# Layer-1 operations at new places in VectorE's and ScalarE's order, and other places for the second layer's weight blocks and three preparations

## The chip, the cores and the metric

One core of one Trainium2 chip. The number is device time in microseconds (us) for one execution; the profile divides that execution into engines: TensorE (PE, with PEld for its weight loads), VectorE (DVE), ScalarE (ACT), GpSimd (POOL) and SyncE (SP, which here only issues DMAs).

## The reference

Attention with a top-32 mask for 4 batches of 8 heads, 576 tokens, 64 numbers a head; then two feed-forward layers of 512 -> 2048 -> 512 over all 2304 tokens, with different activations:

```python
scores = scale * np.matmul(q, k.transpose(0, 1, 3, 2))
kth = np.partition(scores, -32, axis=-1)[..., -32:-31]
scores = np.where(scores >= kth, scores, -1e9)      # then softmax, then times v
# layer 1:  h = x @ w_in;  g = h if h >= 1, 0 if h <= -1, else (h + 1)**2 / 4;  x = g @ w_out
# layer 2:  h = np.maximum(x @ w_in, 0);  out = (h * h) @ w_out
```

## The kernel before

**Slots.** The attention runs in 72 slots, one for each pair of score tiles (128 queries by 576 keys). In slot n VectorE finds the 32nd largest score of each row of both tiles (`rank`): seven operations on each tile, alternately the eight largest (`max`, L920) and their replacement (`match_replace`, L922). `both(op)` issues the pair of one operation, so a slot of VectorE is `both(0)` to `both(6)`. GpSimd masks the tiles of slot n-1 in slot n (`mask`: compare with the threshold, L1083, then multiply, L1088, for each tile). PE computes the scores of slot n+1, turns the masked tiles of slot n-1 (L545) and multiplies them by v; ScalarE copies and exponentiates. VectorE also divides the product with v of slot n-2 by its row sums (`add_to_total` L928, `invert_total` L938, `scale_pv` L948).

**Steps.** The feed-forward work is cut into 18 jobs (a layer and a chunk of 256 tokens) of 16 steps (128 of the 2048 hidden numbers). Steps stand at positions q, three to a slot: q = 3n, 3n+1, 3n+2. Step k at q is `up` (12 matmuls, L613), then a chain: ScalarE's `curve` (L805 to L816), VectorE's `activate` (L977; layer 1 only), ScalarE's `split_g` (L823, L826), called by `hi_at`, GpSimd's `lo_at` (L1101); then PE's `down` at q+2 (L628, L634). The first job starts at q = 31 (slot 10) with two steps a slot; from slot 18 there are three. Jobs of layer 1 hold q 31 to 70, 103 to 168 and 233 to 280; the others are of layer 2. No step stands at q 151 and 152. Slots end with slot 73; from then on the steps run alone.

**Order of work.** Each engine runs a fixed order written out in its `slot(n)`; nothing is reordered at run time. In VectorE's slot `at(3n)` (the job's `split_x`, then `activate`) stands ahead of `both(2)`, `at(3n+1)` ahead of `both(4)`, `at(3n+2)` behind `both(6)`, and behind that VectorE's share of the weight blocks. In ScalarE's slot `hi_at(3n-1)` stands ahead of `curve_at(3n)`. In GpSimd's slot: `mask(n-1, 0)`, `lo_at(3n-1)`, `mask(n-1, 1)`, `lo_at(3n)`, `lo_at(3n+1)`, the preparation of the slot, the slot's weight blocks.

**Weights.** Numbers are held as a high and a low part. A layer has 16 blocks of 128 x 1024. A block lands in a staging buffer by DMA (SP, `stage_block`), ScalarE rounds it to the high part (L694), and GpSimd (L1074) or, for odd blocks of the second layer (`by_vector`), VectorE (L1002) subtracts for the low part. The second layer's blocks are 16 to 31; their slots are given by `W2_PER_SLOT` from slot 19 on. They land in two buffers.

**Preparations.** For each of 16 head pairs, k and q land in `kq_lo` (L324), ScalarE rounds them into `kq_hi` (L686), GpSimd subtracts (L1066), SP stores both (`restack`) and loads them again in another order. `PREP_SLOT` gives the slots. Between slots 17 and 28 `kq_lo` and `kq_hi` hold nothing that is needed, once stored.

Of the kernel before, what the change touches and what calls it, by code (L numbers as in the profile page):

```python
# [33 lines left out]
PREP_ORDER = (2, 3, 0, 1, 4, 5, 6, 7, 8, 9, 10, 11, 12, 13, 14, 15)  # L34
PREP_SLOT = (-1, 1, 3, 5, 7, 10, 12, 15, 17, 28, 30, 32, 38, 41, 44, 47)
WBLOCKS = 16
W_ORDER = [("in", 0)] + [x for j in range(7) for x in (("in", j + 1), ("out", j))] + [("out", 7)]
W1_SLOT = [-1, 0, 0, 1, 2, 2, 3, 4, 4, 5, 6, 6, 7, 8, 8, 9]
W2_PER_SLOT = (1, 2, 2, 1, 2, 2, 1, 2, 2, 1)
W_SLOT = W1_SLOT + \  # L40
# [91 lines left out]
def stage_at(i):  # L132

    return i % 4 if i < WBLOCKS else i % 2


def staged_count(i):

    return i // 4 + 1 if i < WBLOCKS else WBLOCKS // 4 + (i - WBLOCKS) // 2 + 1

# [29 lines left out]
def build(nc, kq, kq0, vv, w_raw, out):  # L170
# [8 lines left out]
    with ctx:  # L179
# [115 lines left out]
        def stage_of(i):  # L295

            return (stage[0], stage[1], xr, ys)[stage_at(i)]

# [12 lines left out]
        def _(sp):  # L311
# [8 lines left out]
            def load_kq(at):  # L320
                g = PREP_ORDER[at]
                if at:
                    sp.wait_ge(restacked, 16 * 3 * at)
                sp.dma_start(kq_lo[:, :].bitcast(F32), kq[g // PAIRS, g % PAIRS]).then_inc(kq_loaded, 16)  # L324

# [54 lines left out]
            def stage_block(i):  # L380
                if i >= WBLOCKS:
                    sp.wait_ge(w_lo_done[i % 2], i // 2)
                elif i >= 4:
                    sp.wait_ge(w_lo_done[i % 2], i // 2 - 1)
                sp.dma_start(stage_of(i)[:, :], w_raw[i]).then_inc(w_staged[stage_at(i)], 16)

# [294 lines left out]
        def _(act):  # L681
# [6 lines left out]
            def split_w(i):  # L688
                s, b = i // WBLOCKS, i % WBLOCKS
                act.wait_ge(w_staged[stage_at(i)], 16 * staged_count(i))  # L690
                if s:
                    wait_block_free(act, s, b)
                    act.wait_ge(w_moved[b], 16)
                act.activation(w_block(b)[:, 0, :], stage_of(i)[:, :], ACT.Copy).then_inc(w_hi_done, 1)  # L694

# [102 lines left out]
            def curve(k):  # L798
# [61 lines left out]
            def slot(n):  # L860
                here, nxt, before = n < SLOTS, n + 1 < SLOTS, 0 <= n - 1 < SLOTS
                q = 3 * n
                if 0 < n <= SIGNED:
                    for t in range(2):
                        keep_by_sign(n - 1, t)
                x_at(n)
                hi_at(q - 1)
                curve_at(q)
                if here:
# [40 lines left out]
        def _(dve):  # L910
# [68 lines left out]

            def at(q):  # L980
                if q in READ_AT:
                    split_x(READ_AT[q])
                if q in UP_AT:
                    activate(UP_AT[q])
# [11 lines left out]
            def split_w(i):  # L996
                if not by_vector(i):
                    return
                dve.wait_ge(w_hi_done, i + 1)
                dve.wait_ge(w_lo_done[i % 2], i // 2)  # L1000
                b = w_block(i % WBLOCKS)
                dve.tensor_tensor(b[:, 1, :], stage_of(i)[:, :], b[:, 0, :].bitcast(F32),  # L1002
                                  ALU.subtract).then_inc(w_lo_done[i % 2], 1)
# [12 lines left out]
            def slot(n):  # L1016
# [6 lines left out]

                both(0)
                if n in (NORMAL, NORMAL + 1):
                    clear_corners(n)
                both(1)
                for c in range(DIRECT):
                    if n == x_slot(c) + 1:
                        split_handed(c)  # L1030
                at(3 * n)
                behind = 1 if n < UP_POS[0] // 3 else 0
                for op in (2, 3, 4):
                    if past and op == 2 + behind:
                        add_to_total(n - 2)
                    if past and op == 3 + behind:
                        invert_total(n - 2)
                    if op == 4:
                        if past and not behind:
                            scale_pv(n - 2)  # L1040
                        at(3 * n + 1)
                    both(op)
                if past and behind:
                    scale_pv(n - 2)
                both(5)
                both(6)
                at(3 * n + 2)
                for i in range(2 * WBLOCKS):
                    if W_SLOT[i] == n:
                        split_w(i)  # L1050
                if n - 1 in SOON:
# [4 lines left out]
            for n in range(SLOTS + 2):  # L1056
                slot(n)
            for q in range(ALONE, END):
                at(q)


        @block.gpsimd
        def _(pool):
# [5 lines left out]
            def split_w(i):  # L1069
                pool.wait_ge(w_hi_done, i + 1)  # L1070
                if i >= 2:
                    pool.wait_ge(w_lo_done[i % 2], i // 2)
                b = w_block(i % WBLOCKS)
                pool.tensor_tensor(b[:, 1, :], stage_of(i)[:, :], b[:, 0, :].bitcast(F32),  # L1074
                                   ALU.subtract).then_inc(w_lo_done[i % 2], 1)
# [126 lines left out]
```

## Time and profile before

Three runs took 1258.48, 1258.61 and 1259.35 us; the median is 1258.61 us.

| | us |
|---|---|
| profiled execution, its own time | 1258.23 |
| its span, first to last instruction | 1256.4 |
| PE busy | 1193.2 (95%) |
| PEld busy | 1128.0 (90%) |
| DVE busy | 851.6 (68%) |
| ACT busy | 799.7 (64%) |
| POOL busy | 749.2 (60%) |

Busy time is the time in which at least one instruction of the engine runs; what an engine waits for inside a slot is read from its instructions in order of time. The granted clock is a share of full speed: 1.00 is 2.4 GHz and 0.50 is 1.2 GHz.

### The profile page before, as it was taken

Reading aid. Unit: us, or ns where it says so; the run is one execution under the profiler, and the core shown is the slowest. Engines: PE = TensorE matmul, PEld = TensorE weight load, DVE = VectorE, ACT = ScalarE, POOL = GpSimd, SP = SyncE. Lnnn points to the kernel's source line nnn. Section 1 sums busy time; section 2 is a strip of 40 time slices with the busy share of each in tenths; the row PEclk is TensorE's granted clock in tenths of the full one; section 3 lists DMA queues with packets and bytes.
Section 4 is the critical chain, followed back from the end, with each engine's and each line's share of the span. In section 5 each row is a group of like instructions: output and inputs, shape, how many; then the busy total and the mean of one; then the engine's idle time right before and its main releaser. Section 6 shows DMA issues by size and latency. Waiting matters only on the chain.

```text
span 1256.4 us, 24445 instructions
## 1 busy us (share of the span) xinstructions
PE 1193.2 (95%) x8760; PEld 1128.0 (90%) x8760; DVE 851.6 (68%) x1884; ACT 799.7 (64%) x1788; POOL 749.2 (60%) x620
## 2 busy tenths in 40 slices
PE   6878889999989999999999999999999999999998
PEld 3667889998889999999999999999999999999997
DVE  7999999999877799999999987868730111110000
ACT  7887666776756666767766665666554665554443
POOL 6767787878767767767666766656652222222222
PEclk9767999999989999999999999999999999999999
DMA  6766978568879932334458831456349300870000
GB/s 250 282 252 223 337 278 301 198 233 301 288 265 367 383 128 97 126 109 142 135 174 299 291 120 39 150 176 208 101 148 369 145 35 4 314 287 18 18 17 17
DMA packets 94920, 239.53 MB, mean 191 GB/s; under 512 B 7760, under 2 KB 46672, under 8 KB 82512
## 3 DMA queue, kind: packets, MB, share of 16 engines
q1 hardware_dynamic: 94800, 237.98, 53.1%
q8 instruction: 70, 1.15, 0.4%
q14 instruction: 50, 0.41, 0.1%
HBM read 166.12 MB, written 71.83 MB: 189 GB/s over the span
## 4 chain that ended last, share of the span: by engine, by line
PE 68%; POOL 12%; DVE 6%; ACT 6%; issue 5%; DMA 1%; SPq 1%; ACTq 0%; POOLq 0%
PE h_ps L613 20%; PE y_ps L634 14%; PE y_ps L628 12%; PE score_ps L613 6%; PE pv_ps L572 5%; POOL s_sb L1083 4%; PE tr_ps L545 4%; POOL prob L1088 4%; DVE top L920 3%; PE score_ps L510 3%; DVE rest L922 2%; POOL w_out L1074 1%; POOL kq_lo L1066 1%; POOL g_lo L1101 1%; PE pv_ps L584 1%
## 5 line engine op out<-in xcount | busy, mean ns | idle before, releaser
L1101 POOL TENSOR_TENSOR g_lo<-rg,g_hi 128x256 fp32r<-128x256 f32 x288 | 215.5, 748 | 407.4 <-ACT g_hi L823 227.9
L613 PE MATMUL h_ps<-xt_hi,w_in 128*128 128x256 f32 x1880 | 390.6, 291 | 2.0 <-DVE xt_lo L968 1.7
L613 PEld LDWEIGHTS h_ps<-xt_hi,w_in 128*128 128x128 f32 x1880 | 309.3, 191 | 4.3 <-issue 2.1
L920 DVE MAX8 top<-rest 128x8 f32<-128x576 f32 x432 | 304.5, 745 | 0.4
L613 PE MATMUL h_ps<-xt_lo,w_in 128*128 128x256 f32 x940 | 266.0, 283 | 0.0
L1083 POOL TENSOR_SCALAR s_sb<-s_sb,top 128x576 f32<-128x576 f32 x126 | 228.2, 1811 | 43.5 <-DVE top L920 43.5
L628 PE MATMUL y_ps<-g_hi,w_out 128*128 128x256 f32 x1152 | 231.8, 284 | 0.7 <-ACT ys L789 0.4
L922 DVE MATCH_REPLACE8 rest<-top,rest 128x576 f32<-128x576 f32 x288 | 211.5, 741 | 0.0
L634 PE MATMUL y_ps<-w_out,g_hi 128*128 128x512 f32 x576 | 203.8, 395 | 3.8 <-DVE w_out L1002 3.1
L1088 POOL TENSOR_TENSOR prob<-s_sb,prob 128x576 f32<-128x576 f32 x128 | 182.7, 1430 | 15.4 <-ACT s_sb L749 4.4
L628 PEld LDWEIGHTS y_ps<-g_hi,w_out 128*128 128x128 f32 x1152 | 189.6, 192 | 2.1 <-issue 0.6
L613 PEld LDWEIGHTS h_ps<-xt_lo,w_in 128*128 128x128 f32 x940 | 180.3, 192 | 1.5
L977 DVE SCALAR_TENSOR_TENSOR rg<-rg 128x256 f32<-128x256 f32 x144 | 83.6, 581 | 134.7 <-ACT rg L816 133.8
L628 PE MATMUL y_ps<-g_lo,w_out 128*128 128x256 f32 x576 | 162.9, 283 | 0.0
L572 PE MATMUL pv_ps<-v_sb,pt 128*128 128x65 f32 x1024 | 132.5, 287 | 0.0
L634 PEld LDWEIGHTS y_ps<-w_out,g_hi 128*128 128x128 f32 x576 | 109.3, 190 | 24.4 <-issue 4.4
L572 PEld LDWEIGHTS pv_ps<-v_sb,pt 128*128 128x128 f32 x1024 | 130.6, 207 | 0.0
L968 DVE TENSOR_TENSOR xt_lo<-xr,xt_hi 128x512 fp32r<-128x512 f32 x32 | 25.1, 826 | 151.2 <-ACT xt_hi L795 151.2
L707 ACT ACTIVATE s_sb<-score_ps 128x576 f32<-128x576 f32 x143 | 92.2, 645 | 55.5 <-PE score_ps L510 28.6
L545 PE MATMUL tr_ps<-ident,prob 128*128 128x128 f32 x576 | 96.2, 293 | 29.0 <-POOL prob L1088 26.9
L805 ACT ACTIVATE rg<-h_ps 128x256 f32<-128x256 f32 x115 | 44.2, 385 | 110.5 <-PE h_ps L613 110.2
L634 PE MATMUL y_ps<-w_out,g_lo 128*128 128x512 f32 x288 | 114.2, 396 | 0.0
(90 smaller groups left out, 2076.1 us busy)
## 6 DMA issues: line engine op xcount, KB each, us to landing
w_in<-w_scratch SPq DMA_DIRECT2D x32, 1024.0 KB, 6.5
w_out<-w_scratch SPq DMA_DIRECT2D x32, 1024.0 KB, 7.9
ks<-kq_scratch SPq DMA_DIRECT2D x46, 576.0 KB, 6.0
qs<-kq_scratch SPq DMA_DIRECT2D x152, 128.0 KB, 4.2
w_scratch<-w_in SPq DMA_DIRECT2D x16, 1024.0 KB, 8.2
w_scratch<-w_out SPq DMA_DIRECT2D x16, 1024.0 KB, 8.1
v_sb<-in_vv_dram SPq DMA_DIRECT2D x48, 325.0 KB, 5.9
stage<-in_w_dram SPq DMA_DIRECT2D x24, 512.0 KB, 4.6
```

The lines of the kernel that those rows point to most:

```text
L545: last = pe.transpose(tr_ps[t][:, P * j:P * (j + 1)], prob[n % 2][:, base + P * j:base + P * (j + 1)], ident[:, :])
L572: last = pe.matmul(pv_ps[:, V1 * t:V1 * (t + 1)], pt[:, base + P * j:base + P * (j + 1)], vb[:, V1 * (2 * j + t):V1 * (2 * j + t + 1)], st ...
L613: last = pe.matmul(h_bank(k), wi[:, f // 2, w, m, cols], x[:, m, :], start=(m == 0 and n == 0), stop=(m == KT - 1 and n == 2))
L628: last = pe.matmul(y_ps[i][:, CHUNK * (m % 2):CHUNK * (m % 2 + 1)], wo[:, f // 2, w, f % 2, P * m:P * (m + 1)], g[f % 2][:, :], start=(f = ...
L634: last = pe.matmul(y_ps[i][:, :], g[f % 2][:, P * i:P * (i + 1)], wo[:, f // 2, w, f % 2, :], start=(f == 0 and n == 0), stop=(f == FT - 1 ...
L707: act.activation(s_sb[u % 4][:, :].rearrange("p (h k) -> p h k", h=2), score_ps[:, :].rearrange("p (h k) -> p h k", h=2)[:, :, 0:HALF], AC ...
L920: dve.max(best, src[:, :]).then_inc(rank_step, 1)
L922: dve.match_replace(rest[t][:, :], best, src[:, :], LOWEST).then_inc(rank_step, 1)
L977: dve.scalar_tensor_tensor(u[:, :], r[:, :], -1.0, u[:, :], ALU.add, ALU.max).then_inc(g_done, 1)
L1083: pool.tensor_scalar(s[:, :], s[:, :], top[n % 2][:, t, TOPK - 1:TOPK], None, ALU.is_ge).then_inc(keep_done, 1)
L1088: pool.tensor_tensor(pr[:, cols], s[:, :], pr[:, cols], ALU.mult).then_inc(masked, 1)
L1101: pool.tensor_tensor(g_lo[k % 2][:, :], g_sb[k % 2][:, :], g_hi[k % 2][:, :].bitcast(F32), ALU.subtract).then_inc(g_lo_done, 1)
```

## The change

- The third step's `activate` (3n+2) moves from the end of VectorE's slot n to behind `both(0)` of slot n+1; the first from ahead of `both(2)` to behind it; the second from ahead of `both(4)` to behind it. `split_x` stays where it was.
- VectorE's low parts of weight blocks move from the end of slot n to behind `both(2)` and `activate(3n)` of slot n+1.
- In slots 2 and 3 the three operations on the product with v stand one pair of `rank` later.
- ScalarE's slot has `curve_at(3n)` ahead of `hi_at(3n-1)`, and `curve` gets a wait on ScalarE's own `split_g` two steps back in layer 2.
- The second layer's 16 blocks take nine slots (19 to 27) where they took ten (19 to 28), and land in four buffers: the two of before, `kq_lo` and `kq_hi`. The preparations of slots 28, 30 and 32 move to 29, 31 and 33. SP waits for the stored pair before it lands a block there, and for all low parts before it loads the next pair.

```diff
-PREP_SLOT = (-1, 1, 3, 5, 7, 10, 12, 15, 17, 28, 30, 32, 38, 41, 44, 47)
+PREP_SLOT = (-1, 1, 3, 5, 7, 10, 12, 15, 17, 29, 31, 33, 38, 41, 44, 47)
+IDLE_KQ = sum(s < 18 for s in PREP_SLOT)
-W2_PER_SLOT = (1, 2, 2, 1, 2, 2, 1, 2, 2, 1)
+W2_PER_SLOT = (1, 2, 2, 2, 2, 2, 2, 2, 1)
 def stage_at(i):
-    return i % 4 if i < WBLOCKS else i % 2
+    return i % 4
 def stage_of(i):
-            return (stage[0], stage[1], xr, ys)[stage_at(i)]
+            if i < WBLOCKS or stage_at(i) < 2:
+                return (stage[0], stage[1], xr, ys)[stage_at(i)][:, :]
+            return (kq_lo, kq_hi)[stage_at(i) - 2][:, 0:2 * MODEL].bitcast(F32)
 def load_kq(at):                      # SP
+                if at == IDLE_KQ:
+                    for i in range(2):
+                        sp.wait_ge(w_lo_done[i], WBLOCKS)
 def stage_block(i):                   # SP
-                if i >= WBLOCKS:
-                    sp.wait_ge(w_lo_done[i % 2], i // 2)
-                elif i >= 4:
+                if i >= 4:
                     sp.wait_ge(w_lo_done[i % 2], i // 2 - 1)
+                if i >= WBLOCKS and stage_at(i) >= 2:
+                    sp.wait_ge(restacked, 16 * 3 * IDLE_KQ)
 def curve(k):                         # ScalarE
                 if k >= 2 and JOBS[(k - 2) // FT][0] == 1:
                     act.wait_ge(g_done, CURVED[k - 2] + 1)
+                elif k >= 2:
+                    act.wait_ge(g_hi_done, k - 1)
 def slot(n):                          # ScalarE
                 x_at(n)
+                curve_at(q)
                 hi_at(q - 1)
-                curve_at(q)
 def slot(n):                          # VectorE
                 both(0)
+                activate_at(3 * n - 1)
                 both(1)
...
-                at(3 * n)
-                behind = 1 if n < UP_POS[0] // 3 else 0
-                for op in (2, 3, 4):
+                read_at(3 * n)
+                behind = 2 if n < RAW_SLOTS else 1 if n < UP_POS[0] // 3 else 0
+                for op in (2, 3, 4, 5, 6):
                     if past and op == 2 + behind:
                         add_to_total(n - 2)
                     if past and op == 3 + behind:
                         invert_total(n - 2)
+                    if past and op == 4 + behind:
+                        scale_pv(n - 2)
                     if op == 4:
-                        if past and not behind:
-                            scale_pv(n - 2)
-                        at(3 * n + 1)
+                        read_at(3 * n + 1)
                     both(op)
-                if past and behind:
-                    scale_pv(n - 2)
-                both(5)
-                both(6)
-                at(3 * n + 2)
-                for i in range(2 * WBLOCKS):
-                    if W_SLOT[i] == n:
-                        split_w(i)
+                    if op == 2:
+                        activate_at(3 * n)
+                        for i in range(2 * WBLOCKS):
+                            if W_SLOT[i] == n - 1:
+                                split_w(i)
+                    if op == 4:
+                        activate_at(3 * n + 1)
+                read_at(3 * n + 2)
```

## Rows read from the trace of the kernel before

**Rows 1.** Busy time by stage: stretch and its length, PE, PEld, DVE, ACT, POOL, PEclk, DMA
```profile
0.00:110.00 110.00, 83.53 (x335) 68.17 (x336) 100.68 (x226) 88.18 (x140) 78.55 (x46) 0.77 0.72 262
110.00:203.10 93.10, 79.42 (x641) 75.17 (x641) 91.00 (x201) 58.46 (x128) 70.97 (x51) 1.00 0.78 295
203.10:371.70 168.60, 157.55 (x1195) 149.72 (x1194) 152.06 (x319) 116.70 (x253) 133.47 (x96) 0.98 0.70 251
371.70:1256.40 884.70, 872.67 (x6595) 834.92 (x6593) 507.89 (x1143) 536.33 (x1268) 466.17 (x430) 1.00 0.45 159
```
**Rows 2.** Waits of the whole span: total us, times, longest
```profile
PE y_ps L634 <- DVE w_out L1002: 3.1, 1, 3.1
PE h_ps L613 <- DVE xt_lo L968: 1.7, 1, 1.7
```
**Rows 3.** Waits of VectorE from 26 to 60 us
```profile
DVE total L928 <- PE pv_ps L572: 1.9, 2, 1.4
```
**Rows 4.** VectorE in order of time, slots 15 to 17: start, duration, [idle before]
```profile
168.11 1.40 DVE L920 MAX8 top<-s_sb 128x8 f32<-128x576 f32 x2
...
174.59 0.76 DVE L977 SCALAR_TENSOR_TENSOR rg<-rg 128x256 f32<-128x256 f32 x1 [0.20 <-ACT rg L816]
...
179.38 1.40 DVE L920 MAX8 top<-s_sb 128x8 f32<-128x576 f32 x2
...
182.15 1.57 DVE L977 SCALAR_TENSOR_TENSOR rg<-rg 128x256 f32<-128x256 f32 x1
...
191.82 0.74 DVE L920 MAX8 top<-s_sb 128x8 f32<-128x576 f32 x1
```
**Rows 5.** GpSimd in order of time, around the start of slot 16
```profile
177.45 2.80 POOL L1066 TENSOR_TENSOR kq_lo<-kq_lo,kq_hi 128x1216 fp32r<-128x1216 f32 x1 [0.36 <-ACT kq_hi L686]
...
182.04 1.40 POOL L1088 TENSOR_TENSOR prob<-s_sb,prob 128x576 f32<-128x576 f32 x1
```
**Rows 6.** ScalarE's first operation of step 3n: slots 21, 22, 27, 28, 30
```profile
243.21 0.39 ACT L810 ACTIVATE rg<-h_ps 128x256 f32<-128x256 f32 x1 [0.21 <-PE h_ps L613]
...
257.95 0.39 ACT L810 ACTIVATE rg<-h_ps 128x256 f32<-128x256 f32 x1 [0.22 <-PE h_ps L613]
...
326.17 0.38 ACT L805 ACTIVATE rg<-h_ps 128x256 f32<-128x256 f32 x1 [2.15 <-PE h_ps L613]
...
339.78 0.38 ACT L805 ACTIVATE rg<-h_ps 128x256 f32<-128x256 f32 x1 [2.28 <-PE h_ps L613]
...
371.67 0.39 ACT L805 ACTIVATE rg<-h_ps 128x256 f32<-128x256 f32 x1 [3.02 <-PE h_ps L613]
```
**Rows 7.** GpSimd in order of time, end of slot 21
```profile
254.58 2.37 POOL L1074 TENSOR_TENSOR w_out<-stage,w_out 128x1024 fp32r<-128x1024 f32 x1 [1.16 <-ACT w_out L694]
256.92 2.95 POOL L1083 TENSOR_SCALAR s_sb<-s_sb,top 128x576 f32<-128x576 f32 x1
```
**Rows 8.** VectorE in order of time, end of slot 21
```profile
257.15 1.21 DVE L1002 TENSOR_TENSOR w_in<-stage,w_in 128x1024 fp32r<-128x1024 f32 x1
```
**Rows 9.** ScalarE's first operation of step 3n in slots 54 and 55
```profile
682.02 0.38 ACT L810 ACTIVATE rg<-h_ps 128x256 f32<-128x256 f32 x1 [1.59 <-PE h_ps L613]
...
694.70 0.39 ACT L810 ACTIVATE rg<-h_ps 128x256 f32<-128x256 f32 x1 [1.59 <-PE h_ps L613]
```
**Rows 10.** VectorE in order of time, slot 54
```profile
683.40 0.43 DVE L977 SCALAR_TENSOR_TENSOR rg<-rg 128x256 f32<-128x256 f32 x1 [0.70 <-ACT rg L816]
```
**Rows 11.** GpSimd in order of time, slot 54
```profile
682.10 0.74 POOL L1101 TENSOR_TENSOR g_lo<-rg,g_hi 128x256 fp32r<-128x256 f32 x1
682.82 1.73 POOL L1083 TENSOR_SCALAR s_sb<-s_sb,top 128x576 f32<-128x576 f32 x1
684.63 1.44 POOL L1088 TENSOR_TENSOR prob<-s_sb,prob 128x576 f32<-128x576 f32 x1
```
**Rows 12.** PE in order of time, slot 54
```profile
687.64 0.60 PE L545 MATMUL tr_ps<-ident,prob 128*128 128x128 f32 x4
```
**Rows 13.** The page's group of the layer-1 high part
```profile
L826 ACT ACTIVATE g_hi<-rg 128x256 fp32r<-128x256 f32 x144 | 60.3, 419 | 64.7 <-DVE rg L977 64.7
```

More of the change, by code:

```diff
@@ L132, in stage_at @@
 def stage_at(i):
-    return i % 4 if i < WBLOCKS else i % 2
-def staged_count(i):
-    return i // 4 + 1 if i < WBLOCKS else WBLOCKS // 4 + (i - WBLOCKS) // 2 + 1
+    return i % 4
 def own_bank(k):
@@ L380, in stage_block @@
             def stage_block(i):
-                if i >= WBLOCKS:
-                    sp.wait_ge(w_lo_done[i % 2], i // 2)
-                elif i >= 4:
+                if i >= 4:
                     sp.wait_ge(w_lo_done[i % 2], i // 2 - 1)
-                sp.dma_start(stage_of(i)[:, :], w_raw[i]).then_inc(w_staged[stage_at(i)], 16)
+                if i >= WBLOCKS and stage_at(i) >= 2:
+                    sp.wait_ge(restacked, 16 * 3 * IDLE_KQ)
+                sp.dma_start(stage_of(i), w_raw[i]).then_inc(w_staged[stage_at(i)], 16)
             def store_block(i):
@@ L689, in split_w @@
                 s, b = i // WBLOCKS, i % WBLOCKS
-                act.wait_ge(w_staged[stage_at(i)], 16 * staged_count(i))
+                act.wait_ge(w_staged[stage_at(i)], 16 * (i // 4 + 1))
                 if s:
@@ L693, in split_w @@
                     act.wait_ge(w_moved[b], 16)
-                act.activation(w_block(b)[:, 0, :], stage_of(i)[:, :], ACT.Copy).then_inc(w_hi_done, 1)
+                act.activation(w_block(b)[:, 0, :], stage_of(i), ACT.Copy).then_inc(w_hi_done, 1)
             def copy_scores(n, t):
@@ L978, in activate, with read_at, activate_at @@
                                              ALU.max).then_inc(g_done, 1)
-            def at(q):
+            def read_at(q):
                 if q in READ_AT:
                     split_x(READ_AT[q])
+            def activate_at(q):
                 if q in UP_AT:
@@ L1001, in split_w @@
                 b = w_block(i % WBLOCKS)
-                dve.tensor_tensor(b[:, 1, :], stage_of(i)[:, :], b[:, 0, :].bitcast(F32),
+                dve.tensor_tensor(b[:, 1, :], stage_of(i), b[:, 0, :].bitcast(F32),
                                   ALU.subtract).then_inc(w_lo_done[i % 2], 1)
@@ L1057, in _ @@
                 slot(n)
+            activate_at(ALONE - 1)
             for q in range(ALONE, END):
-                at(q)
+                read_at(q)
+                activate_at(q)
         @block.gpsimd
@@ L1073, in split_w @@
                 b = w_block(i % WBLOCKS)
-                pool.tensor_tensor(b[:, 1, :], stage_of(i)[:, :], b[:, 0, :].bitcast(F32),
+                pool.tensor_tensor(b[:, 1, :], stage_of(i), b[:, 0, :].bitcast(F32),
                                    ALU.subtract).then_inc(w_lo_done[i % 2], 1)
```

## The prediction

> **What bounds the kernel now.** I read the stages first [rows 1]. Up to 110 us VectorE is busy 100.68 of 110 us and PE 83.53, at a granted clock of 0.77; up to 203.10 us VectorE is busy 91.00 of 93.10 us and PE 79.42 at full clock. There VectorE sets the pace. From 203.10 to 371.70 us, where the second layer's blocks are split, PE is busy 157.55 of 168.60 us and VectorE 152.06: both near full, so what counts is who waits for whom. From 371.70 us to the end PE is busy 872.67 of 884.70 us, and only a wait put in front of PE can change anything. The waits name two direct losses of PE: 3.1 us for VectorE's low part of w_out, 1.7 us for its split of x [rows 2]. Early on VectorE itself waits for the product with v, 1.9 us in two waits [rows 3].
>
> Then slots in order of time. In VectorE's stage a slot without a preparation behind it takes 179.38 - 168.11 = 11.27 us, one with it 191.82 - 179.38 = 12.44 [rows 4]. Where PE leads, a layer-1 slot takes 694.70 - 682.02 = 12.68 us [rows 9]; 257.95 - 243.21 = 14.74 where two weight blocks are split in layer 1, 339.78 - 326.17 = 13.61 in layer 2; and the two slots 28 and 29 take 371.67 - 339.78 = 31.89 us [rows 6].
>
> **Slots 2 and 3.** The operations on the product stand 1.4 us later (one pair, as the MAX8 pair of 1.40 in [rows 4]), so they can take away most of 1.9 us [rows 3]; the product itself doesn't come earlier, and in slot 2 the next scores are close behind. I take 1.4 of a range 0 to 1.9.
>
> **Slots 10 to 18.** In the plain slot the second activate waits 0.20 us for ScalarE and then takes 0.76 us where 0.43 is its undisturbed time [rows 4, 10]: 0.20 + 0.33, so 0.5 us. One pair of rank later ScalarE is done and GpSimd is between two operations, so both go. Slots 10, 12, 14, 15 and 17 gain 0.5 each: 2.6 us. Behind a preparation (slots 11, 13, 16) the first activate takes 1.57 us: it stands behind GpSimd's multiply, which runs to 182.04 + 1.40 = 183.44 [rows 4, 5]. That multiply is late because the preparation before it runs 177.45 to 180.25. After the change the high part of the slot's second step comes 1.4 us later, ScalarE's rounding of the next pair stands behind it, and so the 2.80 us on GpSimd start later too, by some 1.3 us. The multiply, which ended 183.44 - 179.38 = 4.06 us into the slot, then ends at 5.4; the activate, ready at 182.15 - 179.38 = 2.77, is ready one pair later at 4.2, and loses 1.2 again. I take 0 for these three, between -0.3 and +1.1 (1.57 - 0.43) each. In slot 18 PE waits for the same late mask, which gives back some 0.6 of the lead. Sum 2.0 us; range -1 to +6.
>
> **Weight blocks, slots 20 to 27.** Before, GpSimd's block runs 254.58 to 256.95, the compare behind it takes 2.95 instead of 1.73 because VectorE's low part (257.15, 1.21 us) comes ahead of it [rows 7, 8, 11]: 1.2 us. In a two-block slot GpSimd, and ScalarE, which copies both blocks, form a loop: block (2.37), compare, multiply, `lo_at(3n-1)`, compare, multiply (2 x 1.73 + 2 x 1.44 + 0.74 = 7.1), then turn, copies, high part, two block copies and the next block. With the 1.2 us it gives the 14.74 of layer 1. Moved to the middle of the next slot, the low part stands behind `activate(3n)`, which is ready 1.4 us after ScalarE's first operation [rows 9, 10]; GpSimd is then inside that same run of five operations and has no gap. So the 1.2 us stays in layer 1. What changes is how many such slots there are: blocks per slot go from 2, 2, 1, 2 to 2, 2, 2, 2 in slots 20 to 23. One more full slot costs 14.74 - 12.68 = 2.1 us. In layer 2 there is no activate, and by my estimate the low part comes free about 0.6 us after GpSimd's first compare has begun: it waits for the pair ahead of it, 1.4 us, and that for the product with v of two slots before. Does that compare bar it? The rows say no: a compare runs 682.82 to 684.55 and an activate starts at 683.40 and takes its plain 0.43 [rows 10, 11]. So layer 2's full slots stay at about 13.6, less the slots with one block: 0.3 gained over four slots. Sum -1.8 us. Bounds: -5 (the low part collides in layer 2 as well, 4 x 1.2 = 4.8 less 1.6) and +2 (the collision goes in one or two of the layer-1 slots).
>
> A rule of the Trainium skill speaks against this step. "SBUF — State Buffer", section "Who interferes with whom", has it that a VectorE instruction with two SBUF inputs and a GpSimd instruction that reads SBUF shut each other out for the whole instruction, whoever issues first. The multiply of slot 16 bears this out (1.57 us); the compare of slot 54 doesn't, since the activate ran inside it. By the rule the low part would wait for the compare's end in four layer-2 slots, which is rival 4.
>
> **Slots 28 and 29.** Two PE-bound slots take 2 x 12.68 = 25.4 us; they took 31.9 [rows 6, 9], so 6.5 us are lost. The last block (31) was split at the end of slot 28, behind the rounding of a preparation on ScalarE and behind split_x on VectorE, and PE waited 3.1 us for it [rows 2]; after that the clock was down for a while (0.98 over the stage [rows 1]). Now block 31 is rounded in slot 27 and subtracted in the middle of slot 28, some 8 us before `down` at q 87 needs it, and the preparation stands in slot 29. What is late next is split_x for the job that starts at q 87, as at each job start. I leave 0.8 us for it and the preparation in slot 29: 5.7 gained, between 3.1 and 6.5. The preparations at 31 and 33 cost what 30 and 32 cost.
>
> **Landing buffers.** Nothing: no wait of PE is for the staging DMA [rows 2], and GpSimd's block waits for ScalarE [rows 7]. SP's new wait for all low parts stands in front of the load of the tenth pair, needed by ScalarE at the end of the next slot, 12 us on; SP's queue behind it holds loads for two slots ahead. If that cover were gone it would cost up to a landing, some 5 us, which I give no weight.
>
> **From slot 34 on, activate.** VectorE has slack in PE-bound slots (it waits 0.70 us ahead of the activate [rows 10]), so it runs a pair further ahead and the activates stand where they stood against PE. Nothing, except where VectorE was late: at slot 50 PE waited 1.7 us for split_x [rows 2], which stands at the end of VectorE's slot. With an activate less in front, and a pair of lead, it comes 1.3 us earlier. I take 1.5 with a little of the clock; range 0 to 3.2.
>
> **ScalarE's exchange.** This is the term against. `hi_at(3n-1)` now stands behind `curve_at(3n)`. In slot 54 the first operation starts at 682.02 (T); the curve is done at 683.40 - 0.05 (T + 1.35) [rows 9, 10]; the high part overlaps it by 0.1 and takes 0.42 [rows 13], to T + 1.67; GpSimd starts 0.08 later (an estimate, the gap between two of its own operations, 684.63 - 684.55), at T + 1.75. It started at 682.10, T + 0.08. Behind it come 0.74, 1.73, 0.08 between, and 1.44 [rows 11]: the mask of the second tile is ready at T + 5.74 instead of 686.07 (T + 4.05), and PE turns it 0.14 later (an estimate, a little over that gap), at T + 5.88. PE was free for it at 687.64, T + 5.62 [rows 12]. So each PE-bound layer-1 slot that had less than 1.7 us to spare waits 0.26 us. There are 16 of them (35 to 38, 40 to 44, 46, 47, 49, 53 to 55, and 19): 4.2 us. In layer 2 the curve is one operation shorter (T + 0.9), and the same sum ends 0.1 us before PE is free: nothing. Bounds 0 (PE is later than I think) and 8 (twice the wait).
>
> **Sum.** 1.4 + 2.0 - 1.8 + 5.7 + 1.5 - 4.2 = 4.6 us off the profiled 1258.23 us (span 1256.4, and 1.8 around it): 1253.6. The median of the runs stands 0.4 above the profiled one: 1254.0.
>
> **Rivals.**
> 1. ScalarE's exchange costs nothing, because PE takes the turned tiles 0.3 us later anyway, and one prepared slot in three gains its 1.1 us: 4.2 + 1.1 more, 1248.7. For it: the sum is short of the slack by only 0.26 us. Against: it has no gap in it that could shrink. Chance 0.25.
> 2. Slower: the exchange costs more. Not only is the mask late, the copies, the second step's curve and the next `up` follow it, and the six layer-1 slots that carry preparations or job starts pay too: 22 slots. The other terms give 8.8 us, so it decides from 0.40 us a slot; at 0.53 it is 11.7, 2.9 slower: 1261.5. For it: in slot 54 all these stand on one chain. Against: the rows give 0.26. Chance 0.14.
> 3. The change doesn't do at slot 28 what it says: PE's 3.1 us pass to split_x, which waits for the last `up` of the job on ScalarE, and the preparation of slot 29 meets it. 1 us instead of 5.7: 1258.7. For it: split_x stands ahead of block 31 in VectorE's order, so part of the 3.1 us may be its own. Against: 2.3 us of ScalarE's copies leave slot 28. Chance 0.10.
> 4. The low part waits for the whole compare in layer 2: 1.1 us (1.73 - 0.6) more in four slots, 4.4: 1258.4. Against: [rows 10, 11] as above. Chance 0.09.
>
> **How the numbers follow.** My forecast has 0.42. 0.2% is 2.5 us, about what can be told from no change: faster is below 1256.1, slower above 1261.1. The forecast's own spread puts 0.36 of its 0.42 below 1256.1; with 0.25 of rival 1 and 0.05 of rivals 3 and 4 that is 0.66. Slower: 0.12 of rival 2 and 0.02 elsewhere, 0.14. Same 0.20. Range 1247.5 to 1261.0: rival 1 with a microsecond of VectorE's stage on one side, nearly all of rival 2 on the other.
>
> **What would show it.** The first MAX8 of slot 18 some 3 to 4 us before 203.10; the plain slot at 10.7 instead of 11.27, the one behind a preparation still 12.4. Slots 21 to 23 at 14.7 each, the compare or `lo_at` lengthened by 1.2. No wait of PE for L1002, slots 28 and 29 together near 26. Steady layer-1 slots at 12.94 instead of 12.68, with PE waiting for L1088 ahead of the second L545; if they stay at 12.68 that term is wrong. I am wrong as a whole if the 31.89 doesn't shrink, or if layer-1 slots lengthen by 0.4 or more.

## The result, and the profile after

The changed kernel takes 1266.06 us in the median of 4 runs (1265.70 to 1267.39), the kernel before 1258.55 (4 runs): ratio 1.0063, 95% interval 1.0051 to 1.0075. It is 7.5 us slower; 4.6 faster was forecast. The profiled execution has a span of 1264.3 us (1256.4 before), so 7.9 us stand in the trace to be found. One of the five executions of d1 (below) took 1447.5 us at a mean granted clock of 0.76; it isn't counted, and its profile isn't used.

The stages, cut at the same times as [rows 1], in the same columns:

```profile
0.00:110.00 110.00, 83.44 (x326) 68.13 (x326) 101.43 (x228) 88.33 (x141) 78.77 (x47) 0.76 0.73 263
110.00:203.10 93.10, 83.66 (x659) 80.93 (x659) 89.77 (x202) 57.28 (x129) 70.23 (x50) 0.96 0.79 294
203.10:371.70 168.60, 158.04 (x1194) 149.40 (x1193) 151.19 (x320) 117.52 (x256) 131.40 (x95) 0.99 0.69 248
371.70:1264.30 892.60, 873.84 (x6585) 831.86 (x6585) 505.20 (x1137) 531.45 (x1264) 468.22 (x431) 1.00 0.45 159
```

The last stage is 7.9 us longer, but PE is busy only 1.2 us more in it: what was added is waiting. (The cut is at one time for both kernels. The changed one reaches ScalarE's slot 30 2.2 us earlier, at 369.44 us instead of 371.67, so from that slot on it loses 10.1 us.) The waits of PE over the whole span name whom for:

```profile
PE tr_ps L546 <- POOL prob L1096: 27.0, 29, 4.8
...
PE y_ps L635 <- POOL g_lo L1109: 2.4, 3, 1.4
...
PE y_ps L629 <- POOL g_lo L1109: 1.5, 2, 1.2
PE tr_ps L546 <- POOL prob L1102: 1.5, 2, 1.0
```

The two waits of [rows 2] are gone, as forecast. In their place stand 3.9 us for `g_lo`, the low part that GpSimd makes of the layer output (it had 0.3 us before), and a new 1.5 us for a mask (L1102). The 27.0 us for the other masks look like the 26.9 of before, but hide a shift: behind 230 us they rose from 9.3 to 13.2 us.

VectorE against [rows 3] (26 to 60 us) and [rows 4] (slots 15 to 17):

```profile
DVE total L931 <- PE pv_ps L573: 0.3, 1, 0.3
```

```profile
167.24 1.40 DVE L923 MAX8 top<-s_sb 128x8 f32<-128x576 f32 x2
171.40 0.41 DVE L980 SCALAR_TENSOR_TENSOR rg<-rg 128x256 f32<-128x256 f32 x1
...
177.88 1.40 DVE L923 MAX8 top<-s_sb 128x8 f32<-128x576 f32 x2
182.04 1.47 DVE L980 SCALAR_TENSOR_TENSOR rg<-rg 128x256 f32<-128x256 f32 x1
...
190.29 0.73 DVE L923 MAX8 top<-s_sb 128x8 f32<-128x576 f32 x1
```

The plain slot fell from 11.27 to 10.64 us, the one behind a preparation stayed at 12.41, with an activate of 1.47 us (1.57 before).

ScalarE's first operation of step 3n in slots 21, 22, 23, 24, 28 and 30, against [rows 6]. I call the time from one of these to the next slot's "stretch n":

```profile
242.94 0.38 ACT L813 ACTIVATE rg<-h_ps 128x256 f32<-128x256 f32 x1 [2.23 <-PE h_ps L614]
257.57 0.38 ACT L813 ACTIVATE rg<-h_ps 128x256 f32<-128x256 f32 x1 [2.23 <-PE h_ps L614]
272.20 0.38 ACT L813 ACTIVATE rg<-h_ps 128x256 f32<-128x256 f32 x1 [2.23 <-PE h_ps L614]
289.70 0.38 ACT L808 ACTIVATE rg<-h_ps 128x256 f32<-128x256 f32 x1 [2.54 <-PE h_ps L614]
...
343.02 0.38 ACT L808 ACTIVATE rg<-h_ps 128x256 f32<-128x256 f32 x1 [3.53 <-PE h_ps L614]
...
369.44 0.38 ACT L808 ACTIVATE rg<-h_ps 128x256 f32<-128x256 f32 x1 [2.56 <-PE h_ps L614]
```

Stretches 21 and 22 are the forecast 14.6, stretch 23 is 17.5, and 28 and 29 together are 26.42 instead of 31.89.

Slot 54, against [rows 9 to 12]: ScalarE with the next slot's first operation, GpSimd, PE.

```profile
683.80 0.38 ACT L813 ACTIVATE rg<-h_ps 128x256 f32<-128x256 f32 x1 [3.53 <-PE h_ps L614]
...
685.05 0.40 ACT L829 ACTIVATE g_hi<-rg 128x256 fp32r<-128x256 f32 x1
...
696.72 0.38 ACT L813 ACTIVATE rg<-h_ps 128x256 f32<-128x256 f32 x1 [3.53 <-PE h_ps L614]
```

```profile
685.53 0.73 POOL L1109 TENSOR_TENSOR g_lo<-rg,g_hi 128x256 fp32r<-128x256 f32 x1 [2.27 <-ACT g_hi L829]
686.25 1.73 POOL L1091 TENSOR_SCALAR s_sb<-s_sb,top 128x576 f32<-128x576 f32 x1
688.06 1.44 POOL L1096 TENSOR_TENSOR prob<-s_sb,prob 128x576 f32<-128x576 f32 x1
```

```profile
688.89 0.70 PE L511 MATMUL score_ps<-ks,qs 128*128 128x288 f32 x4
689.64 0.63 PE L546 MATMUL tr_ps<-ident,prob 128*128 128x128 f32 x4
```

The same matmuls ahead of the turn, before (the turn itself is [rows 12]):

```profile
687.11 0.69 PE L510 MATMUL score_ps<-ks,qs 128*128 128x288 f32 x4
```

With T = 683.80, `lo_at(3n-1)` starts at T + 1.73, the mask ends at T + 5.70 and PE turns it at T + 5.84 (forecast: 1.75, 5.74, 5.88). The turn starts 0.75 us after the scores ahead of it, 0.53 before: that is 0.22 of the loss, though the view prints no idle time there. The stretch is 12.92 us, +0.24 on [rows 9], forecast +0.26. So the steady slot is right, and most of the loss is elsewhere.

Stretches in us, one trace each, of the kernels named below; "first 20" is the time of ScalarE's first operation of step 3n in slot 20:

```
           before  changed     a1     a4     d2     d4     e2     e1
first 20   230.27   230.02 230.97 230.80 230.74 230.14 230.19 229.59
21 + 22     29.48    29.26  29.27  29.46  29.44  27.81  29.28  27.80
23          12.66    17.49  17.65  15.29  12.66  12.66  13.13  12.66
24          14.02    12.80  12.80  14.33  14.02  14.25  14.73  14.26
28 + 29     31.89    26.42  25.39  25.38  26.28  31.20  26.38  26.29
30 to 34    64.62    66.38  65.96  65.97  65.97  64.59  65.97  65.97
36          12.66    12.91  12.67  12.67  12.67  12.67  12.67  12.67
50 to 52    36.85    35.85  34.63  35.76  36.84  34.63  34.65  34.65
56          11.55    13.06  11.56  11.56  11.55  11.56  11.56  11.56
71          12.97    14.14  12.98  12.98  12.98  12.99  12.97  12.98
72          10.75    12.98  10.76  10.76  10.76  10.76  10.76  10.76
```

### The profile page after: what moved, and what is told of

Its sections match the earlier page's. It is cut to its first block, busy times and chain, and to the rows that moved or that the text cites. A ratio compares the mean times of both kernels' runs of the same rounds, so it can differ in the third digit from the quotient of the medians.

```text
span 1264.3 us, 24596 instructions
## 1 busy us (share of the span) xinstructions
PE 1199.0 (95%) x8760; PEld 1130.3 (89%) x8760; DVE 847.6 (67%) x1884; ACT 794.6 (63%) x1788; POOL 748.6 (59%) x620
## 4 chain that ended last, share of the span: by engine, by line
PE 55%; POOL 18%; DVE 12%; issue 8%; ACT 6%; DMA 1%; ACTq 0%; SPq 0%; POOLq 0%
PE h_ps L614 16%; PE y_ps L629 10%; PE y_ps L635 10%; POOL s_sb L1091 7%; PE score_ps L614 6%; DVE top L923 5%; PE pv_ps L573 5%; POOL prob L1096 4%; DVE rest L925 4%; POOL g_lo L1109 3%; PE tr_ps L546 3%; PE score_ps L511 2%; POOL prob L1099 1%; POOL kq_lo L1074 1%; DVE rg L980 1%
## 5 line engine op out<-in xcount | busy, mean ns | idle before, releaser
L1091 POOL TENSOR_SCALAR s_sb<-s_sb,top 128x576 f32<-128x576 f32 x126 | 223.2, 1772 | 15.8 <-DVE top L923 15.8
L1096 POOL TENSOR_TENSOR prob<-s_sb,prob 128x576 f32<-128x576 f32 x128 | 186.8, 1462 | 15.3 <-DVE top L923 3.1
L980 DVE SCALAR_TENSOR_TENSOR rg<-rg 128x256 f32<-128x256 f32 x144 | 77.7, 540 | 138.7 <-ACT rg L819 138.3
L808 ACT ACTIVATE rg<-h_ps 128x256 f32<-128x256 f32 x115 | 44.2, 384 | 127.2 <-PE h_ps L614 126.9
L813 ACT ACTIVATE rg<-h_ps 128x256 f32<-128x256 f32 x120 | 46.0, 383 | 122.7 <-PE h_ps L614 117.2
```

The source lines that it names most:

```text
L980: dve.scalar_tensor_tensor(u[:, :], r[:, :], -1.0, u[:, :], ALU.add, ALU.max).then_inc(g_done, 1)
L1091: pool.tensor_scalar(s[:, :], s[:, :], top[n % 2][:, t, TOPK - 1:TOPK], None, ALU.is_ge).then_inc(keep_done, 1)
L1096: pool.tensor_tensor(pr[:, cols], s[:, :], pr[:, cols], ALU.mult).then_inc(masked, 1)
```

## The experiments

### Which part costs: the exchange, VectorE's order, the schedule

**a1**: the change without ScalarE's exchange (its added wait in `curve` stays).

```diff
-                curve_at(q)
                 hi_at(q - 1)
+                curve_at(q)
```

> The changed kernel with ScalarE's exchange undone: hi_at(3n-1) stands ahead of curve_at(3n) again, all else as changed. Theory A (the exchange is the largest loss): the 0.25 us of each steady layer-1 slot (about 3.7 in all), 1.5 at slot 56, 3.4 at slots 71 to 73 and some 1 in slots 62 to 70 come back, 9 to 10 us: 1256.5, steady layer-1 slots at 12.67. Theory B (VectorE's new order loses them, the exchange only the 0.25 a slot): 3.7 back, 1262.3, and slots 71 to 73 stay long.

Measured 1254.23 us (5 runs), ratio 0.9965 [0.9952, 0.9978]: 11.8 us under the changed kernel, more than either theory. The exchange alone turns a faster kernel into a slower one.

**a2**: the kernel before with the exchange alone, and the wait that it needs.

```diff
+                elif k >= 2:
+                    act.wait_ge(g_hi_done, k - 1)
...
+                curve_at(q)
                 hi_at(q - 1)
-                curve_at(q)
```

> The kernel before with the exchange on ScalarE alone (and the wait that it needs). Theory A: the same losses as in the changed kernel, plus more in slots 20 to 28 where the mask is late already: 9 to 11 us, 1268.5. Theory B: 0.25 us in some 16 slots, 1262.5.

1269.61 us (4 runs), 1.0090 [1.0075, 1.0105]: +10.7 us over 1258.93. It costs about as much with and without the rest: from slot 20 on the traces give 10.8 us here and 12.2 between a1 and the changed kernel. Stretches 29, 56, 71 and 72 lengthen by the same 1.0, 1.5, 1.2 and 2.2 us in both; 34 and 50 do not (1.1 against 0.4, and -0.7 against +1.3).

**a3**: the change with VectorE's low parts back at the end of the slot.

```diff
                     if op == 2:
                         activate_at(3 * n)
-                        for i in range(2 * WBLOCKS):
-                            if W_SLOT[i] == n - 1:
-                                split_w(i)
...
                 read_at(3 * n + 2)
+                for i in range(2 * WBLOCKS):
+                    if W_SLOT[i] == n:
+                        split_w(i)
```

> The changed kernel with VectorE's low parts of weight blocks back at the end of the slot in which ScalarE rounds the block. Theory A (slot 23 lost 4.3 us because the low part met GpSimd in the middle of the slot, just ahead of split_x): slot 23 falls from 17.5 us to 15 or less, 2.5 to 4 us back: 1262.8. Theory B (slot 23 is long because two blocks are rounded ahead of the last curve, wherever the low part stands): slot 23 stays at 17, 1266, or 1267 with VectorE later.

1267.44 us (4 runs), 1.0064 [1.0047, 1.0081]: the total of B. Stretch 23 fell to 14.48, as A said, and 24 rose from 12.80 to 18.30: nothing gained. Stretches 22 to 24 sum to 46.7 us, 44.9 in the changed kernel and 41.4 before: the debt only moves.

**a4**: the new preparations, blocks and landing buffers, with both engines' orders of before.

> The kernel before with only the new schedule: nine slots of blocks, four landing buffers, preparations at 29, 31, 33; VectorE's and ScalarE's orders as before. Theory A (the schedule is good for 6 us at slots 28 and 29 and costs 2 to 3 at slots 22 to 24): 1255 to 1256. Theory B (the third full slot costs 4 us under any order): 1257 to 1258.5, no gain.

1255.95 us (8 runs), 0.9980 [0.9970, 0.9991], as A: 6.5 us won in stretches 28 and 29, 2.9 lost in 22 to 24. The landing buffers, the blocks and the preparations were not run apart.

**d4**: the counterpart, VectorE's new order alone, low parts at the end of the slot.

> The kernel before with VectorE's new order of layer 1 and of the product alone (slots 2 and 3 too; the low parts of the weights at the end of the slot, ScalarE's order, landing buffers and preparations as before). My prediction's terms: 1.4 for slots 2 and 3, 2.0 for slots 10 to 18, 1.5 at slot 50, 4.9 in all, 1253.7. Theory A (a1 and a4 have the same span, so it is worth nothing but slot 50): 1257.5, slot 18's first MAX8 at 202 to 203. Theory B (the terms add): 1254.

1254.66 us (7 runs), 0.9970 [0.9960, 0.9981]: the total of B, by other terms. First 20 is only 0.13 us earlier. 1.67 us come from stretches 21 and 22, 0.7 from 28, 2.2 from 50 to 52.

### Where the exchange costs

The trace of the changed kernel at slot 56, ScalarE, GpSimd and PE:

```profile
709.70 1.16 ACT L796 ACTIVATE xt_hi<-xr 128x512 fp32r<-128x512 f32 x2 [3.59 <-PE h_ps L614]
710.75 0.37 ACT L813 ACTIVATE rg<-h_ps 128x256 f32<-128x256 f32 x1
...
711.99 0.40 ACT L829 ACTIVATE g_hi<-rg 128x256 fp32r<-128x256 f32 x1
```

```profile
712.46 0.73 POOL L1109 TENSOR_TENSOR g_lo<-rg,g_hi 128x256 fp32r<-128x256 f32 x1 [3.37 <-DVE top L923]
```

```profile
713.25 0.39 PE L629 MATMUL y_ps<-g_hi,w_out 128*128 128x256 f32 x1 [1.24 <-POOL g_lo L1109]
```

A job starts here, and `curve_at(3n)` begins with split_x of its input (L796): ScalarE waits for the last `up` of the job before (3.59 us of idle time), rounds x for 1.16 us, and the high part of step 3n-1 is behind it. In the kernel before, GpSimd began that low part at 707.45 us, 1.04 ahead of the slot's first curve operation (708.49); now it begins at 712.46, 1.71 behind it (710.75), and PE's `down` stands still. Slots 34 and 72 are built alike: there PE waits 0.85 and 1.36 us for the low part.

**e3** undoes the exchange in these three slots.

```diff
+HI_FIRST = (34, 56, 72)
...
+                if n in HI_FIRST:
+                    hi_at(q - 1)
                 curve_at(q)
-                hi_at(q - 1)
+                if n not in HI_FIRST:
+                    hi_at(q - 1)
```

> The changed kernel with ScalarE's exchange undone in three slots alone, 34, 56 and 72, where split_x of a new job stands at the head of curve_at(3n). Theory A (there PE's `down` waits for the low part, which stands behind split_x and the curve): stretches 34, 56 and 72 go back from 12.51, 13.06 and 12.98 us to about 12.1, 11.55 and 10.76, and all else stays: 4.2 us off, 1261.9. Theory B (the slots behind them are late by the same chain and keep the loss): under 2 us off, 1264 or more.

Stretches 34, 56 and 72 are 12.07, 11.56 and 10.74 us: 4.2 us back, as A; stretches 23 and 68 take 0.4 of it, and 3.8 arrive at the end. The total, 1263.31 us (4 runs), 1.0037 [1.0023, 1.0051], is only 2.8 under the changed kernel. In the trace first 20 stands at 230.90 us, 0.9 later, though no instruction differs up to slot 33 (see the last section).

**c3** has HI_FIRST = (29, 34, 35, 50, 51, 56, 61, 67, 71, 72).

> The changed kernel with ScalarE's exchange undone in ten slots alone: 29, 34, 35, 50, 51, 56, 61, 67, 71 and 72, those that lengthened by another amount than the 0.25 us of the steady ones. Theory A (the exchange costs two things that add up: 0.25 us in each steady slot, and some 8 us in these ten): 7 to 8 us off, 1258.5. Theory B (one chain: what these ten give back is lost again in the slots behind them): 2 to 4 us off, 1263.

1258.49 us (10 runs), 1.0002 [0.9992, 1.0012], span 1256.5: 7.6 us back, as A. The ten stretches cost 8.3 us in the changed kernel against a1, and c3's trace is 8.2 us shorter from slot 20 on. The costs are local and add up.

**c1** keeps the exchange and moves GpSimd's low part.

```diff
-                lo_at(q - 1)
+                if n not in MASK_FIRST:
+                    lo_at(q - 1)
                 if before:
                     mask(n - 1, 1)
+                if n in MASK_FIRST:
+                    lo_at(q - 1)
```

> The changed kernel, with one thing put in another order on GpSimd: in slots 36, 37, 38, 41, 43, 44, 46, 47, 49, 53 to 56, 71 and 72 the low part of the step before (lo_at(3n-1)) stands behind the second tile's mask instead of ahead of it. ScalarE's exchange stays. Theory A (the mask stands in GpSimd's queue behind a low part that waits for the late high part): the steady slots among them go from 12.92 back to 12.67 us, slot 56 from 13.06 to about 11.6, slot 72 falls by 1 us or more; in all 13 x 0.25 + 1.5 + 1 to 2 = 6 to 7 us off, 1259.5. Theory B (the cost is the second step's curve, which comes later on ScalarE, or the late high part itself, for which `down` waits): the slots stay where they are, 1265 to 1266.

1266.40 us (4 runs), 1.0067 [1.0052, 1.0082]: the total of B, the slots of both. (Its trace has first 20 1.3 us later than the changed kernel; from there on it is 1.1 us shorter.) Steady stretches of the list (36 to 38, 54) are 12.67 us again, while 42, which isn't in it, keeps 12.91. So there the mask behind the late low part is the whole cost; in stretch 71, 13.27 us instead of 14.14, it is most of it. But stretch 56 rose to 13.32 and 72 to 14.90, because there PE waits for the low part itself, which now comes later still. The wait of PE in stretch 72:

```profile
930.94 0.50 PE L636 MATMUL y_ps<-w_out,g_hi 128*128 128x512 f32 x1 [2.36 <-POOL g_lo L1110]
```

It was 1.36 us in the changed kernel. One edit, two mechanisms that ask for opposite orders on GpSimd.

### Slots 22 to 24

Stretch 23 of the changed kernel: GpSimd, VectorE, PE, then two stretches of time in the columns of [rows 1] (the granted clock is the third number from the end).

```profile
275.43 2.69 POOL L1091 TENSOR_SCALAR s_sb<-s_sb,top 128x576 f32<-128x576 f32 x1
278.20 2.51 POOL L1096 TENSOR_TENSOR prob<-s_sb,prob 128x576 f32<-128x576 f32 x1
```

```profile
274.78 1.75 DVE L1007 TENSOR_TENSOR w_in<-stage,w_in 128x1024 fp32r<-128x1024 f32 x1
...
278.17 1.28 DVE L971 TENSOR_TENSOR xt_lo<-xr,xt_hi 128x512 fp32r<-128x512 f32 x2
```

```profile
280.86 0.63 PE L546 MATMUL tr_ps<-ident,prob 128*128 128x128 f32 x4 [2.10 <-POOL prob L1096]
```

```profile
278.00:281.40 3.40, 1.30 (x11) 1.04 (x10) 3.40 (x9) 1.79 (x5) 3.32 (x3) 1.00 1.04 424
281.40:284.80 3.40, 3.31 (x16) 3.05 (x15) 3.40 (x7) 2.96 (x5) 1.28 (x3) 0.50 0.98 283
```

The low part stands against the compare (2.69 us, 1.73 elsewhere), split_x of the job at q 71 against the multiply (2.51, 1.43 elsewhere). PE is busy 1.30 of 3.40 us, and behind that its granted clock is 0.50 (1.2 GHz) up to 284.8 us. My "one more full slot costs 2.1 us" held for 21 and 22 and not where a full slot meets a job start.

**c2** took a block out of slot 23, and was a mistake of mine: what slot n issues shows in stretch n + 1.

```diff
-W2_PER_SLOT = (1, 2, 2, 2, 2, 2, 2, 2, 1)
+W2_PER_SLOT = (1, 2, 2, 2, 1, 2, 2, 2, 2)
```

> The changed kernel with ScalarE's exchange undone (a1) and slot 23 splitting one block instead of two, slot 27 two instead of one. Theory A (the third full slot in a row is what the 17.6 us of slot 23 are made of): slot 23 falls to 14 us or less, slots 27 and 28 rise by 1 to 1.5 us, net 2 to 3 us off a1: 1251.7. Theory B (a debt of the weight work that is only moved): slots 24 to 28 take up what slot 23 gives, 1253.5 to 1254.5.

1255.26 us (9 runs), 0.9975 [0.9966, 0.9985]; stretch 23 at 17.39 and 28 at 14.91. It is neither theory's result: nothing was gained in 23, and 28 paid 1.0 us for the block that it got.

**d1** and its repeat **e2** take it out of slot 22.

```diff
+W2_PER_SLOT = (1, 2, 2, 1, 2, 2, 2, 2, 2)
```

> The changed kernel with ScalarE's exchange undone (a1) and one weight block instead of two issued in slot 22 (blocks per slot from 19: 1, 2, 2, 1, 2, 2, 2, 2, 2). What a slot issues shows in the stretch that begins with the next slot's first operation, so c2, which took the block out of slot 23, took it out of the wrong one. Theory A (17.65 us of stretch 23 are the third full slot in a row meeting split_x of the job that starts at q 71): stretch 23 falls to 13 us or less, stretch 24 rises from 12.80 to about 14, stretch 28 rises by 1; net 2.5 us off a1, 1251.7. Theory B (the low part in the middle of the slot meets split_x, one block or two): stretch 23 stays over 15, total within 1 us of a1, 1254.

> d1 again, for its profile at full clock: the changed kernel with ScalarE's exchange undone and one block in slot 22. Theory A (third full slot in a row): stretches 23 and 24 fall from 17.65 + 12.80 us to about 12.7 + 14.2, stretch 28 rises from 13.89 to 14.9. Theory B (it is the low part's place in the middle of the slot that meets split_x): stretch 23 stays over 15. Total as d1, 1252.7.

1252.46 us (4 runs), 0.9956 [0.9942, 0.9970], and 1252.63 (4 runs), 0.9954 [0.9940, 0.9967]. The stretches are e2's: 23 is 13.13, 24 is 14.73, 28 rose by 1.0. That is A's mechanism, at 1.6 us net instead of 2.5, since 24 rose by 1.9. Whether the full slot at the job start must be the third in a row was not tested: no run has one alone there. **d2**, the same number in a4:

> The orders of before with the change's places for the preparations, its landing buffers, and one block in slot 22 (a4 with that one number). Theory A: stretches 22 to 24 go from 44.35 us back to 41.4 as before, stretch 28 rises by 1, 2 us off a4: 1253.9. If VectorE's new order is worth nothing here either, it ends as d1 does, within 1 us. Theory B: nothing, 1256.

1253.56 us (5 runs), 0.9961 [0.9948, 0.9975], stretches 22 to 24 at 41.41 as before and 28 up by 0.9, as A.

### VectorE's stage

**c4**: slots 2 and 3 alone, on the kernel before.

```diff
-                behind = 1 if n < UP_POS[0] // 3 else 0
+                behind = 2 if n < RAW_SLOTS else 1 if n < UP_POS[0] // 3 else 0
```

> The kernel before with one part of the change: in slots 2 and 3 VectorE's three operations on the product with v stand one pair of rank later. Theory A (the waits of 1.9 us go and the lead is kept): 1.4 us off, 1257.2 against 1258.6. Theory B (the slots 4 to 6 are bound by ScalarE and GpSimd and take the lead back): 1258.3 to 1258.9, with slot 7 beginning at most 0.5 us earlier.

1259.36 us (10 runs), 1.0007 [0.9998, 1.0017], as B: VectorE's slot 4 begins at 47.25 us instead of 48.56, slot 7 at 78.81 instead of 78.47.

**d3**: a1 with VectorE's second activate a pair of rank earlier again.

> The changed kernel with ScalarE's exchange undone (a1) and VectorE's second activate of a slot put back ahead of the fifth pair of rank. Theory A (in the slots behind a preparation it is this activate, a pair late, that lengthens the chain high part, rounding, preparation): VectorE's slots 13 and 16 fall from 13.54 and 13.23 to about 12.5, the plain slots rise from 10.64 by 0.5, and slot 18 starts within 0.5 us of a1's 202.53; total 1253.5 to 1255. Theory B (VectorE waits 2.8 us there for ScalarE's second curve, and only waits sooner): slots 13 and 16 stay over 13.2 while the plain slots rise, total 1256 to 1257.

1257.12 us (10 runs), 0.9991 [0.9982, 1.0000]. Slots 13 and 16 fell to 12.78 and 12.65 as A says; the plain slots rose to 11.45, each with 0.72 us of waiting, and the total is that of B. What the new order gains in the plain slots it gains by this second activate: without it they are longer than before (11.27). The price of the later place is a1's longest wait of VectorE, in slot 13:

```profile
154.25 0.43 DVE L980 SCALAR_TENSOR_TENSOR rg<-rg 128x256 f32<-128x256 f32 x1 [2.79 <-ACT rg L819]
```

### The version that beats both

**e1**: VectorE's new order with low parts at the slot's end, the new preparations and buffers, one block in slot 22, no exchange.

> VectorE's new order with the weights' low parts at the end of the slot (d4), the change's preparations and landing buffers, one block in slot 22 (d2), ScalarE's order as before. d4 stands 4.0 us under before, d2 5.1. Theory A (they add, less what both take at VectorE's stage and in stretches 28 to 34): first operation of slot 24 at 283.5 us as in d4, stretches 28 and 29 together 26.3 as in d2, stretches 50 and 51 22.1 as in d4; 1250.5. Theory B (they share one gain, as a1 and a4 had the same span): 1253 as d2.

1249.66 us (5 runs), 0.9932 [0.9918, 0.9945]: 9.2 us under before, as A. Stretches 21 and 22 are 13.90 us each; the trace shows why, GpSimd and then VectorE at the end of slot 21:

```profile
253.05 2.58 POOL L1082 TENSOR_TENSOR w_out<-stage,w_out 128x1024 fp32r<-128x1024 f32 x1 [1.16 <-ACT w_out L695]
255.60 1.90 POOL L1091 TENSOR_SCALAR s_sb<-s_sb,top 128x576 f32<-128x576 f32 x1
```

```profile
252.18 1.21 DVE L1007 TENSOR_TENSOR w_in<-kq_hi,w_in 128x1024 fp32r<-128x1024 f32 x1
```

With a pair of lead, the low part at the slot's end meets the start of GpSimd's block instead of the compare: the block takes 2.58 us against 2.37, the compare 1.90 against 2.95 [rows 7, 8].

## Why the prediction was wrong

The sum was to be -4.6 us and is +7.9 (both against the profiled execution). Term by term, from the table and the same stretches (before, a1 and the changed kernel):

```
                          forecast  measured   miss
slots 2 to 18 (first 20)     -3.4     -0.25    +3.1
weight blocks, 20 to 27      +1.8     +3.6     +1.8
slots 28 and 29              -5.7     -6.5     -0.8
preparations at 31 and 33     0       +1.3     +1.3
slots 50 to 52               -1.5     -2.2     -0.7
exchange, from slot 20       +4.2    +12.2     +8.0
the rest                      0       -0.3     -0.3
```

- **Exchange, the step that failed.** "Each PE-bound layer-1 slot that had less than 1.7 us to spare waits 0.26 us. There are 16 of them" is right as a sum: they cost 3.9 us together, most 0.25 each (35 and 46 cost 0.5, 44 gained 0.3). "In layer 2 ... nothing", and no price for slots that start a job, is wrong: of the 12.2 us, 6.0 stand in the stretches of layer 2 (24 to 34 and 57 to 72). I took `curve_at(3n)` for three operations of 1.35 us (by my own rows 683.35 - 682.02 = 1.33, which changes nothing). At q 102, 168 and 216 it holds split_x too, with a wait for PE ahead of it: 0.44 + 1.51 + 2.21 = 4.2 us, given back by e3. The other 4.3 us stand in 29, 50, 71 and a few more, and c3 gives back most of them. In the changed kernel PE waits for the mask there, 1.09 us at 362.28, 1.06 at 640.85 and 1.05 at 921.19. For 71 c1 shows that it is the mask behind the late low part; why these slots have less room than the steady ones stays open.
- **Rival 1**, no cost at all, is out with the steady slots. **Rival 2** named the exchange as the danger and priced it at 11.7 us; it cost that, but as some 0.25 in each steady slot and 8.3 us in ten others (from -0.6 to +2.2), not as 22 times 0.53. I gave it 0.14.
- **VectorE's stage.** Slots 2 and 3 did win 1.5 us where I said, and slots 4 to 6 took 1.0 back; c4 shows that nothing arrives. Slots 10 to 17 won 1.6 of 2.0, and VectorE's slot 18 begins 1.9 us earlier (201.16 against 203.10). PE doesn't get it. GpSimd's preparation at the end of slot 17 begins only 0.5 us earlier, and PE, at the turn in stretch 18, waits longer for the mask behind it. GpSimd and PE of the changed kernel, then the same two of before:

```profile
200.69 2.78 POOL L1074 TENSOR_TENSOR kq_lo<-kq_lo,kq_hi 128x1216 fp32r<-128x1216 f32 x1 [0.37 <-ACT kq_hi L687]
...
206.81 0.63 PE L546 MATMUL tr_ps<-ident,prob 128*128 128x128 f32 x4 [1.04 <-POOL prob L1096]
```

```profile
201.16 2.78 POOL L1066 TENSOR_TENSOR kq_lo<-kq_lo,kq_hi 128x1216 fp32r<-128x1216 f32 x1 [0.37 <-ACT kq_hi L686]
...
207.30 0.63 PE L545 MATMUL tr_ps<-ident,prob 128*128 128x128 f32 x4 [0.47 <-POOL prob L1088]
```

  That is the chain (high part, rounding, preparation, mask) at which I let "some 0.6 of the lead" go; it and the exchange's 0.25 in slot 19 took 1.7 of the 1.9 us. The mean over the ten traces with the whole new order says the same: 1.6 us ahead at VectorE's slot 18, 0.1 at first 20 (229.59 to 231.55, against 230.27 to 230.80 of before, a4, d2 and c4, which has the new places in slots 2 and 3 alone). I counted a lead of VectorE as time of the kernel without following the chain that hands it to PE.
- **Weight blocks.** 14.6 for stretches 21 and 22 and "the 1.2 us stays in layer 1" hold (compare 2.69, so 1.0). Slot 23 is the error. In layer 2, stretches 25 to 27 changed by 0.1 us in sum, so rival 4 is out; the changed kernel around the start of stretch 25 shows the low part inside the compare, both at their plain length:

```profile
301.69 1.72 POOL L1091 TENSOR_SCALAR s_sb<-s_sb,top 128x576 f32<-128x576 f32 x1
```

```profile
302.42 1.21 DVE L1007 TENSOR_TENSOR w_in<-stage,w_in 128x1024 fp32r<-128x1024 f32 x1
```

- **Slots 28 and 29.** Right (5.7 forecast, 5.5 in the changed kernel, 6.5 without the exchange), so rival 3 is out. But "the preparations at 31 and 33 cost what 30 and 32 cost" was short by one: the preparation now in slot 29 shows as 1.3 us in stretch 30; before it was hidden in the 31.9.
- **Slot 50.** Right: PE no longer waits 1.7 us for split_x, and d4 shows that VectorE's order alone gives the 2.2 us.

## What to carry to other kernels

Before an engine's two steps are exchanged, list every instruction that the moved-ahead step can contain in any slot, with its waits; the rare slot where it starts a job cost up to nine times the steady one (2.21 us against 0.25). A stall taken away on the busiest engine counts only as far as the chain through the other engines comes earlier too. And an edit of three parts is worth splitting: here one part's 12 us hid 9 us that the others, put right, were worth.

## What the hardware showed

- VectorE's and GpSimd's operations lengthen each other, and how much depends on where in the operation they meet. VectorE first: a low part that starts 0.65 us before the compare makes it 2.69 us instead of 1.73, split_x 0.03 before the multiply makes that 2.51 instead of 1.43. GpSimd first: an activate 0.1 to 0.2 us into the multiply takes 1.47 to 1.57 us instead of 0.41. In a compare it is barred for a part only. Those that start 0.09, 0.31, 0.41 and 0.58 us into it take 0.94, 0.71, 0.61 and 0.43: all end 1.01 to 1.03 us into it, so they are held until it has run for 0.6 of its 1.73 us, and later ones take their plain 0.40 to 0.43. One pair from the kernel before:

```profile
654.79 1.73 POOL L1083 TENSOR_SCALAR s_sb<-s_sb,top 128x576 f32<-128x576 f32 x1 [2.17 <-DVE top L920]
```

```profile
655.20 0.61 DVE L977 SCALAR_TENSOR_TENSOR rg<-rg 128x256 f32<-128x256 f32 x1
```

  "SBUF — State Buffer", section "Who interferes with whom", in the Trainium skill bars the second engine for the whole instruction. The multiply agrees; the compare agrees for its first 0.6 us only, and layer 2's stretches didn't lengthen by what that rule would cost. The start times alone don't always say who goes first: the low part of [rows 8] starts 0.23 us into the compare of [rows 7], straight behind an activate that had waited for GpSimd's block, and it is the compare that is longer (2.95).
- The same instructions can take different courses. Up to slot 20 a1, c2 and e2 are one program, and stretch 13 is 13.68, 13.09 and 12.95 us, first 20 at 230.97, 229.89 and 230.19. The changed kernel, c1, c3 and e3, alike up to slot 28, have first 20 between 230.02 and 231.28; c1 and c3 ran on one chip and differ by 0.8. A term under 1 us in this stage can't be read from one trace.
- The granted clock before 110 us was 0.76 in the changed kernel and 0.95 in a1, whose first 20 is later nonetheless. In this stage, where VectorE is busy 101 of 110 us, these traces show no cost of the slower PE above the 1 us by which they differ anyway.
